# A convolution and two MLPs in fp32r parts: the down projection's low products one pair later

## What is computed

```
w = softmax(weight)                      # 8 heads x 7 taps
x = causal_conv(x, w)                    # (16384, 192)
h = relu(x @ moe_w_in)                   # (16384, 2048)
x = (h * h) @ moe_w_out                  # (16384, 192)
h = x @ moe2_w_in
g = where(h > 0, h, exp(min(h, 0)) - 1)  # ELU
out = g @ moe2_w_out                     # (16384, 192)
```

## Time and profile before

| | |
|---|---|
| median of 3 runs | 2257.91 us |
| the profiled execution | 2258.32 us |
| its span | 2256.5 us |
| TensorE, matmuls busy | 2218.7 us (98%), 19456 matmuls |
| TensorE, weight loads busy | 1824.8 us (81%) |
| VectorE busy | 1751.2 us (78%) |
| ScalarE busy | 1546.8 us (69%) |
| GpSimd busy | 45.9 us (2%), all in the first 78 us |
| share of TensorE in the chain that ended last | 97% |
| granted TensorE clock, mean | 0.999 |

### The profile page before, as it was taken

How to read it: one execution, slowest core, us unless ns; L and a number is a source line. 1 busy time by engine, 2 the same in 40 slices (tenths; PEclk the granted TensorE clock), 3 DMA queues, 4 the chain that set the end, 5 groups by cost and what they waited for, 6 DMA issues and landing times.

```text
span 2256.5 us, 50993 instructions
## 1 busy us (share of the span) xinstructions
PE 2218.7 (98%) x19456; PEld 1824.8 (81%) x19456; DVE 1751.2 (78%) x2903; ACT 1546.8 (69%) x2826; POOL 45.9 (2%) x36
## 2 busy tenths in 40 slices
PE   5999999999999999999999999999999999999998
PEld 3788888888888888888888888888888888888887
DVE  7787777787777877777877778777778777787777
ACT  4666677766677666777666776667776677676675
POOL 5300000000000000000000000000000000000000
PEclk9999999999999999999999999999999999999999
DMA  4210111101111101111011111011110111110101
GB/s 113 72 32 26 33 40 31 40 24 30 35 35 35 30 26 33 40 31 40 18 35 35 31 40 30 26 33 40 31 38 18 33 40 31 40 30 24 35 21 29
DMA packets 80821, 79.22 MB, mean 35 GB/s; under 512 B 5024, under 2 KB 70560, under 8 KB 80800
## 3 DMA queue, kind: packets, MB, share of 16 engines
q1 hardware_dynamic: 80800, 78.93, 13.6%
HBM read 24.39 MB, written 12.58 MB: 16 GB/s over the span
## 4 chain that ended last, share of the span: by engine, by line
PE 97%; DVE 1%; ACT 1%; DMA 0%; issue 0%; SPq 0%; DVEq 0%; ACTq 0%
PE bank_h L274 46%; PE bank_a L291 20%; PE bank_a L311 10%; PE bank_b L311 10%; PE bank_b L291 10%; DVE conv_b L460 0%; DVE act_lo L502 0%; DVE conv_a L460 0%; DMA x_cols<-in_x_dram 0%; ACT act_hi L377 0%; DMA mov_s<-mov_a 0%; ACT relu L372 0%; ACT act L382 0%; DVE conv_b L457 0%; DVE mov_a L465 0%
## 5 line engine op out<-in xcount | busy, mean ns | idle before, releaser
L502 DVE TENSOR_TENSOR act_lo<-act,act_hi 128x512 fp32r<-128x512 f32 x1024 | 687.4, 695 | 305.6 <-ACT act L382 285.5
L291 PE MATMUL bank_a<-act_hi,down 64*128 64x512 f32 x4096 | 621.7, 387 | 1.1 <-DVE sum_a L483 0.7
L393 ACT CAST act_hi<-act 128x512 fp32r<-128x512 f32 x512 | 318.6, 622 | 339.2 <-DVE act L510 338.0
L291 PEld LDWEIGHTS bank_a<-act_hi,down 64*128 64x128 f32 x4096 | 384.1, 185 | 82.4 <-ACT act_hi L393 1.2
L372 ACT ACTIVATE relu<-bank_h 128x512 f32<-128x512 f32 x512 | 278.6, 597 | 227.5 <-PE bank_h L274 227.5
L311 PE MATMUL bank_a<-act_lo,down 64*128 64x512 f32 x2048 | 404.3, 391 | 6.6 <-DVE act_lo L502 6.4
L311 PE MATMUL bank_b<-act_lo,down 64*128 64x512 f32 x2048 | 399.7, 387 | 0.0
L291 PE MATMUL bank_b<-act_hi,down 64*128 64x512 f32 x2048 | 389.3, 387 | 0.0
L510 DVE TENSOR_TENSOR act<-bank_h,expo 128x512 f32<-128x512 f32 x512 | 354.1, 692 | 17.5
L388 ACT ACTIVATE expo<-bank_h 128x512 f32<-128x512 f32 x512 | 278.0, 595 | 106.0 <-PE bank_h L274 103.3
L274 PE MATMUL bank_h<-mov_a,up_hi 64*128 64x512 f32 x2048 | 317.3, 388 | 24.0 <-DMA mov_s<-mov_a 24.0
(11 more groups left out here) (45 smaller groups left out, 1690.4 us busy)
## 6 DMA issues: line engine op xcount, KB each, us to landing
mov_s<-mov_a SPq DMA_DIRECT2D x128, 256.0 KB, 3.4
x_cols<-in_x_dram SPq DMA_DIRECT2D x32, 536.0 KB, 4.3
mov_b<-mov_b SPq DMA_DIRECT2D x32, 256.0 KB, 4.2
out_dram<-sum_a SPq DMA_DIRECT2D x32, 256.0 KB, 2.7
out_dram<-out_b SPq DMA_DIRECT2D x32, 128.0 KB, 2.4
raw_down<-in_moe_w_out_dram SPq DMA_DIRECT2D x16, 192.0 KB, 3.2
raw_up<-in_moe_w_in_dram SPq DMA_DIRECT2D x16, 128.0 KB, 3.4
raw_up<-in_moe_w_in_dram SPq DMA_DIRECT2D x16, 64.0 KB, 3.2
```

What stands on the lines that cost most here:

```text
L291: pe.matmul(bank[:, :], down[kind[h]][rows, f, cols], act_hi[s][rows, :], start=first and t == 0 and n == 0, stop=False)
L393: act.copy(act_hi[s][:, :], act32[s][:, :]).then_inc(hi_ready, 1)
L502: dve.tensor_tensor(act_lo[s][:, :], act32[s][:, :], act_hi[s][:, :].bitcast(F32), ALU.subtract)\
```

## The change

TensorE does the low products of pair q - 1 behind the high products of pair q; in the last pair of each half both pairs' low products come at the end. So step q = 0 of a half has no low products. `down_done` is split into two semaphores, `hi_read` (high products of a pair done) and `lo_read` (low products done). ScalarE's `reuse` now waits for `hi_read` and for `lo_ready` of the pair before the last; VectorE's `lo_part` waits for `lo_read` before it overwrites `act_lo`. In ELU halves VectorE makes pair 0's low parts only after pair 1's `elu`. In the very last pair TensorE does the low products of pair 6 before the high products of pair 7, and of pair 7's low products those into `bank_b` first; ScalarE then copies `bank_b` before `bank_a`, and VectorE adds b before a.

```diff
-            def down_project(b, kind, h, q):
+            def down_hi(b, kind, h, q):
...
-                hi_products(1, (HI_LO_B,), bank_b)
-                for t in range(2):
-                    f, s = q + PAIRS * t, 2 * (q % 2) + t
-                    w, lo, stop = down[kind[h]], act_lo[s], last and t == 1
+                hi_products(1, (HI_LO_B,), bank_b).then_inc(hi_read, 1)
+
+            def lo_products(kind, h, q, t, cols, banks):
+                f, s = q + PAIRS * t, 2 * (q % 2) + t
+                for rows, bank in zip(ROWS, banks):
+                    done = pe.matmul(bank[:, :], down[kind[h]][rows, f, cols], act_lo[s][rows, :],
+                                     start=False, stop=q == PAIRS - 1 and t == 1)
+                return done
+
+            def down_lo(b, kind, h, q):
+
+                before = STEPS * (2 * b + h) + 2 * q
+                for t in range(2):
                     pe.wait_ge(lo_ready, before + t + 1)
-                    for cols, banks in ((HI_A, bank_a), (HI_LO_B, bank_b)):
-                        for rows, bank in zip(ROWS, banks):
-                            done = pe.matmul(bank[:, :], w[rows, f, cols], lo[rows, :], start=False, stop=stop)
-                done.then_inc(down_done, 1)
+                    lo_products(kind, h, q, t, HI_A, bank_a)
+                    done = lo_products(kind, h, q, t, HI_LO_B, bank_b)
+                done.then_inc(lo_read, 1)
+
+            def very_last_lo(b, kind, h, q):
+
+                before = STEPS * (2 * b + h) + 2 * q
+                for t in range(2):
+                    pe.wait_ge(lo_ready, before + t + 1)
+                    done = lo_products(kind, h, q, t, HI_LO_B, bank_b)
+                done.then_inc(last_b_done, 1)
+                for t in range(2):
+                    done = lo_products(kind, h, q, t, HI_A, bank_a)
+                done.then_inc(lo_read, 1)
...
-                        down_project(b, kind, h, q)
+                        very_last = kind == END and h == 1 and q >= PAIRS - 2
+                        if not very_last:
+                            down_hi(b, kind, h, q)
+                            if q > 0:
+                                down_lo(b, kind, h, q - 1)
+                            if q == PAIRS - 1:
+                                down_lo(b, kind, h, q)
+                        elif q == PAIRS - 2:
+                            down_hi(b, kind, h, q)
+                            down_lo(b, kind, h, q - 1)
+                        else:
+                            down_lo(b, kind, h, q - 1)
+                            down_hi(b, kind, h, q)
+                            very_last_lo(b, kind, h, q)
...
-                act.wait_ge(down_done, PAIRS * (half + 1))
+                act.wait_ge(lo_read, PAIRS * (half + 1))
...
-                    act.wait_ge(down_done, pairs_before(b, h) + q - 1)
+                    act.wait_ge(hi_read, pairs_before(b, h) + q - 1)
+                    act.wait_ge(lo_ready, 2 * (pairs_before(b, h) + q - 1))
...
+            act.wait_ge(last_b_done, 1)
+            copy_b(2 * LAST + 1)
             copy_a(2 * LAST + 1)
-            copy_b(2 * LAST + 1)
             copy_b_lo(2 * LAST + 1)
...
             def lo_part(b, h, q, t):
                 s = 2 * (q % 2) + t
+                if t == 0 and not (isinstance(b, int) and b == 0 and h == 0 and q < 2):
+
+                    dve.wait_ge(lo_read, pairs_before(b, h) + q - 1)
...
                             for t in range(2):
                                 elu(b, h, q, t)
                             bank_sums(b, kind, h, q)
-                            for t in range(2):
-                                lo_part(b, h, q, t)
+                            if q == 1:
+                                for t in range(2):
+                                    lo_part(b, h, 0, t)
+                            if q > 0:
+                                for t in range(2):
+                                    lo_part(b, h, q, t)
...
+            add_b(2 * LAST + 1)
             add_a(2 * LAST + 1, 1)
-            add_b(2 * LAST + 1)
```

More of the change, by code:

```diff
@@ L117, in bass_conv_mlp_mlp_kernel @@
         lo_ready = sem("lo_ready")
-        down_done = sem("down_done")
+        hi_read = sem("hi_read")
+        lo_read = sem("lo_read")
+        last_b_done = sem("last_b_done")
         part_a_done = sem("part_a_done")
@@ L276, in up @@
                 done.then_inc(h_ready, 1)
-            def down_project(b, kind, h, q):
+            def down_hi(b, kind, h, q):
                 half, before = 2 * b + h, STEPS * (2 * b + h) + 2 * q
-                first, last = q == 0, q == PAIRS - 1
+                first = q == 0
                 used = first and not (kind == FIRST and h == 0)
@@ L290, in hi_products @@
                         for rows, bank in zip(ROWS, banks):
-                            pe.matmul(bank[:, :], down[kind[h]][rows, f, cols], act_hi[s][rows, :],
-                                      start=first and t == 0 and n == 0, stop=False)
+                            done = pe.matmul(bank[:, :], down[kind[h]][rows, f, cols], act_hi[s][rows, :],
+                                             start=first and t == 0 and n == 0, stop=False)
+                    return done
                 pe.wait_ge(hi_ready, before + 1)
```

## The result

The changed kernel takes 2270.89 us, the median of 6 runs (2269.03 to 2272.25), against 2258.3 for the kernel before (6 runs, 2257.11 to 2259.38). The ratio is 1.0056, with an interval of 1.0046 to 1.0066: 12.6 us slower, where 11.5 were forecast. The profiled execution has a span of 2269.6 us, 13.1 more than before.

What follows compares the result with a forecast made beforehand. TensorE was taken as the bound, busy 2100.00 of 2100.00 us. The terms -5.1 + 19.5 - 0.9 - 2.0 = +11.5 us gave a median forecast of 2269.4 us, range 2257 to 2278 for 8 in 10.

Steps and rivals of the forecast that it cites:

- The wait removed: Step q = 0 of 32 ELU halves: low products no longer wait for act_lo, 32 x 0.16 = -5.1 us.
- Pair 2 late: ELU halves: pair 2's second high products 0.50 us late plus 0.11 weight load, 32 x 0.61 = +19.5 us.
- The added waits at nothing: VectorE's added lo_read wait and ScalarE's new reuse waits cost nothing; otherwise 0.05 per VectorE operation or 0.1 a half.
- The weight load behind each gap: The slot behind a late product pays an unhidden weight load, 0.11 us (0.34 less 0.23).
- The start: Program's first halves: the step of pair 0's high products ends as if at 77.8 instead of 78.73, -0.9 us.
- one such stretch again, which stands in the count above: At the start, idling brings one 1.2 GHz stretch again (1.7 us of work), covered since TensorE waits for mov_b anyway.
- The end: Last pair and final stores: -0.91 - 1.05 = -1.96 us.
- The 0.91 of the last pair: In the last pair, high products' waits for casts, with the slots behind them 0.91 us in all, go.
- the 1.05 of the store's issue: bank_b's copy starts 0.94 earlier and sum_b gains 0.11, bringing out_b's store 1.05 us sooner.
- 1: VectorE catches up and no pair is late in any half: 2249.9 us, chance 0.07.
- 2: Only ScalarE's path binds in the ELU halves, +5.4 us instead of +19.5: 2255.3 us, chance 0.15.
- Rival 3: Low stalls remain as act_lo comes later too: 2274.5 us, with other lateness up to 2282; chance 0.10.

Runs made afterwards that it cites:

- e10: Kernel before, TensorE's order and end untouched, with b's sums and the input's split later and the first half's mov_b copy behind pair 6: 2255.67 us, ratio 0.9994.
- e2: Changed kernel with mid_b's sum moved to q = 4 in the looped ELU halves and the next input's split two pairs later: 2252.24 us, ratio 0.9979.
- e1: Changed kernel with mid_b's sum moved from q = 1 to q = 4 in the 30 looped ELU halves: 2257.95 us, ratio 1.0003.
- e4: Changed kernel with one more 0.61 us VectorE operation right behind mid_b's sum in the 30 looped ELU halves: 2289.32 us, ratio 1.0141.
- e9: Changed kernel with only the split of the next input moved two pairs later, mid_b's sum left in place: 2271.36 us, ratio 1.0062.
- e3: Changed kernel with pair 0's low parts made with q = 0 again, before pair 1's elu, in ELU halves: 2282.83 us, ratio 1.0113.
- e8: Kernel before with only the end changed: last pair's low products into bank_b first, b copied and summed before a: 2256.19 us, ratio 0.9994.
- e7: Changed kernel with mid_b's sum and input split later, first half's mov_b copy behind pair 6, last tile's b sums at q = 2 and 4: 2247.53 us, ratio 0.9956.
- e5: Changed kernel with TensorE's old order of low products in the program's first half alone: 2269.44 us, ratio 1.0053.

## Why the prediction was right, point by point

**The wait removed: -5.1.** Right. No wait for act_lo is left between 80 and 2180, and e10, with the old order, still has it. The old ELU half was 34.65 long; without gaps (e2) it is 34.48, 0.17 less where 0.16 was forecast.

**Pair 2 late: +19.5.** Right in place, cause and size. The chain was forecast step by step from T as 2.87, 5.00, 7.40, 8.01 and 10.93, and measured as 2.88, 5.01, 7.41, 8.01 and 10.92. The gaps of a looped half add up to 0.59 (0.61 forecast), the net is 0.42 a half and 13.1 for 31 halves. e1, e4 and e9 show the cause: mid_b's 0.61 taken out of VectorE's queue gives back 0.42, where ScalarE's path then binds as forecast (0.17 left), 0.61 put in costs 0.61, and ScalarE's copy alone gives nothing.

**The added waits at nothing.** Right: four act_lo take 2.48 us for all (0.60 each), though the first of each two waits for lo_read as well. In e2 the added waits of both engines stand as in the changed kernel, and no gap is left in its looped ELU halves; its ReLU halves are 34.45 long, as in the kernel before.

**The weight load behind each gap: 0.11.** 0.112 and 0.110 measured. TensorE's queue did not load the weights of the next slot across the wait, and leaving the 0.11 in the sum was right.

**The start: -0.9.** Wrong in sign: +0.86 in the profiled pair, about +1 by the profiles together. The stand for act_hi until 62.72 and the wait for mov_b's low part until 68.4 came as forecast, and the sum_a wait did go (77.33 follows 9 slots behind 75.29, with no gap). The step that failed is "one such stretch again, which stands in the count above": the clock stayed at 1.2 GHz through the wait for mov_b and for most of the up products behind it, whose slots took 0.43 us (68.44 to 71.9). The half ended at 75.3, where 73.5 was forecast: 3.3 us at half the clock cost 1.6 of these 1.8. I had listed a second low stretch in the upper bound (+1.7) and taken -0.9. Which of the two comes is not fixed by the code. In e2, e3 and e9 the low stretch was over (66.2 to 68.0) before the up products started (68.5 to 68.8), and the half ended at 73.8 to 74.2, near the forecast; in the changed kernel, e1 and e4 it was not, and the half ended at 75.3 to 75.6.

**The end: -1.96.** The 0.91 of the last pair went whole (the half got about 0.45 longer by pair 2's gap less the old wait, and still ended up 0.44 shorter), and the 1.05 of the store's issue came to 0.01. But 0.65 was lost after it; I had named the two stores' hindering each other as a possible loss of half, and e8 shows that stores just as close together land in 2.4, so the loss does not come from their closeness; what it comes from is open.

Sum: the loop 0.9 lower than forecast (13.5 with the END halves), the start 1.8 higher, the end 0.65 higher: +13.1 in the spans, against 11.5. That the total came so near is in part luck: the loop's miss and those of the start and the end have opposite signs, and the start's changes from one execution to the next.

**Rivals.** 1 and 2 asked for pair 2 in time or nearly; e2 and e1 are what they describe, in the looped halves. They come out at 0.9979 and 1.0003, where the rivals' 2249.9 and 2255.3 would be 0.9965 and 0.9988: about 3 us higher each. The start and the store's landing (1.8 and 0.65 over the forecast in the changed kernel) and the gaps that stay in the two END halves are of that size. Rival 3 did not happen: act_lo of pair 0 is ready in time.

## What to carry to other kernels

Taking work out of the first step of a stage brings forward the due time of all that the other engines do for the following steps. Before moving it, add up each in-order queue between the release of the second step's input and the third's result, and compare with the new due time; here 0.2 us to spare and the 0.4 that VectorE made up could not pay for a due time 1.1 sooner. Work with no near due time (mid_b, made at 1229.60 and first read at 1267.85, or the next input's split) is what to move out of that stretch, and each engine's queue must be counted, since the shortened one only passes the bound to the next (e1 to e2, and e3).

## What the runs showed of the hardware

- A late product of TensorE costs more than its lateness: the next slot starts 0.337 instead of 0.227 us behind it, in every repeated gap of the looped halves of the ten kernels that have one (e2 and e7 have none).
- In the six profiles with the changed kernel's start, the granted clock fell while TensorE stood still for 5.7 us (until 62.72 in the changed kernel). It was low for 10.2 us in the changed kernel, e1 and e4, and for 6.8 in e2, e3 and e9, with the same code at the start. That makes the same start 1.1 to 1.8 us longer or shorter between executions. With TensorE's old order there it was low for 3.4 us each time: behind the wait for act_lo in the kernel before (62.9 to 66.3), and earlier, between 52.9 and 58.3, in e5, e8 and e10. The Trainium skill's page "TensorE: Matmul & The Clock Gate" (HAM oscillation) says that idling brings the half clock back; the trace agrees (0.64 of full between 63 and 75).
- VectorE's pitch for fp32 operations with two inputs of 512 columns that don't depend on the one before is 0.60 us, with 0.69 in the records; waits on two or three semaphores that are met by then don't lengthen it (act_lo at 1227.20, and at 77.33, 0.60 behind sum_b at 76.73).
